# An attention and feed-forward kernel on one core: raw keys and queries loaded once, a third place for the maxima's operands, casts a head sooner

## The reference

```
scores = q @ k.T / 8;  cum = cumsum(maximum(s, 0))
scores = where(j > i, -1e9, scores + minimum(cum[j] - cum[i], 0))
attn   = softmax(scores);  x = attn @ v               # heads side by side: 512 wide
h = relu(x @ w_in)                                    # 512 -> 1024
h = h * sigmoid(conv3(h));  x = h @ w_out             # 3 taps along the positions
u = x + (U @ V mixes the positions of x)              # rank 32
out = u + relu(u @ w_ch1) @ w_ch2                     # 512 -> 2048 -> 512
```

## Time and profile before

| what | value |
|---|---|
| median of 3 runs | 897.69 us (897.37 to 901.75) |
| profiled execution, its own time | 895.65 us |
| its span | 893.8 us |
| PE busy | 852.6 us (95%) |
| DVE busy | 465.5 us (52%) |
| ACT busy | 377.6 us (42%) |
| DMA | 150.36 MB, mean 168 GB/s |
| body 0, attention alone | to about 79 us |
| PE from 820 to 840 us, dense products alone | 153 in 20.00 us, 0.131 each |

### The profile page before, as it was taken

How to read it: one execution, slowest core, us unless ns; L and a number is a source line. 1 busy time by engine, 2 the same in 40 slices (tenths; PEclk the granted TensorE clock), 3 DMA queues, 4 the chain that set the end, 5 groups by cost and what they waited for, 6 DMA issues and landing times.

```text
span 893.8 us, 15677 instructions
## 1 busy us (share of the span) xinstructions
PE 852.6 (95%) x6184; PEld 803.2 (90%) x6184; DVE 465.5 (52%) x976; ACT 377.6 (42%) x717; POOL 50.8 (6%) x105
## 2 busy tenths in 40 slices
PE   4888999989999999999999999999999999999998
PEld 3666889879999899999999999999999999999998
DVE  6788686465447925554444951555323732442222
ACT  2777665553426624554233643444222631221110
POOL 3021000000000000000000000000000000000000
PEclk9999999999999999999999999999999999999999
DMA  6686847638563547536535544435435433364441
GB/s 163 168 231 156 289 128 242 219 72 255 199 206 125 175 156 246 176 112 208 168 137 172 175 129 166 135 131 161 149 142 178 166 141 143 142 223 161 168 162 54
DMA packets 64396, 150.36 MB, mean 168 GB/s; under 512 B 30026, under 2 KB 44362, under 8 KB 51780
## 3 DMA queue, kind: packets, MB, share of 16 engines
q1 hardware_dynamic: 61252, 144.50, 49.2%
q0 software_dynamic: 3072, 4.87, 2.0%
HBM read 119.15 MB, written 30.11 MB: 167 GB/s over the span
## 4 chain that ended last, share of the span: by engine, by line
PE 76%; DVE 12%; ACT 6%; issue 4%; DMA 1%; SPq 1%; DVEq 0%; ACTq 0%; POOL 0%
PE psum L1208 21%; PE psum L1210 20%; PE psum L1209 20%; PE psum L1187 6%; DVE psum L916 2%; PE psum L1134 2%; PE psum L1166 2%; PE psum L1164 2%; DVE work L978 2%; DVE work L981 2%; DVE qb L903 1%; ACT work L760 1%; PE psum L1147 1%; PE psum L1274 1%; PE psum L1171 1%
## 5 line engine op out<-in xcount | busy, mean ns | idle before, releaser
L1208 PE MATMUL psum<-uu_hl,ring 128*128 128x288 f32 x512 | 153.0, 299 | 2.4 <-DVE uu_hl L1016 1.5
L1208 PE MATMUL psum<-r_hl,ring 128*128 128x288 f32 x512 | 153.0, 299 | 0.0
L1210 PE MATMUL psum<-r_hl,ring 128*128 128x288 f32 x512 | 151.2, 295 | 0.0
L1209 PE MATMUL psum<-r_hl,ring 128*128 128x288 f32 x512 | 151.1, 295 | 0.0
L1210 PE MATMUL psum<-uu_hl,ring 128*128 128x288 f32 x512 | 150.9, 295 | 0.0
L1209 PE MATMUL psum<-uu_hl,ring 128*128 128x288 f32 x512 | 150.8, 294 | 0.0
L797 ACT ACTIVATE r_hl<-psum 128x288 fp32r<-128x288 f32 x128 | 52.4, 410 | 179.9 <-PE psum L1210 179.8
L1021 DVE SCALAR_TENSOR_TENSOR r_hl<-psum,r_hl 128x288 fp32r<-128x288 f32 x128 | 58.2, 457 | 134.3 <-ACT r_hl L797 134.2
L1187 PE MATMUL psum<-probs,va 128*65 128x320 f32 (+4 forms) x448 | 107.8, 360 | 7.6 <-ACT probs L699 7.6
L916 DVE CUSTOM_DVE_ANT_0 psum<-psum,key_late 128x512 f32<-128x512 f32 (+4 forms) x160 | 84.7, 564 | 46.5 <-PE psum L1134 45.4
L1033 DVE TENSOR_TENSOR u_acc<-psum,u_acc 128x288 f32<-128x288 f32 x96 | 43.8, 457 | 115.5 <-PE psum L1210 115.5
(11 more groups left out here) (102 smaller groups left out, 1616.0 us busy)
## 6 DMA issues: line engine op xcount, KB each, us to landing
...
```

What stands on the lines that cost most here:

```text
L1208: pe.matmul(o, hi, m_hi, start=start, stop=False)
L1209: pe.matmul(o, hi, m_lo, start=False, stop=False)
L1210: return pe.matmul(o, lo, m_hi, start=False, stop=stop)
```

## The change

What it does:

- The raw keys and queries are loaded once, to partitions 0 to 63. Partition 64 of `kq_raw` holds the rows of sums; the tensor `sums` is gone; `s` is read into `work`.
- `qc` has three buffers too. ACT casts straight into `kc` and `qc` (semaphore `cast`), and `max_scores` waits for these. In body 0 and head (1, 0), listed in ALONE, it does so in step 1, else in steps 2 and 3.
- `kb` and `qb` hold the second copy of the high part and the low part, in exchanged halves. For n = 1 to 10 DVE makes the second copy (`key_parts`, `query_parts`); for others ACT, in steps 0 and 1 of the head before (`second_keys`, `second_queries`).
- In body 0 the heads 0, 2, 4, 6 put their values at another place of PSUM (`out_at`), and the eviction of head h comes in step 0 of head h + 1, between its exponentials. `values` waits for the eviction of n - 2.
- The splits of pairs 0 and 1 of batch 0 go from heads 5 and 7 to head (1, 0); pair 2's normalise and split move by a step.
- Weight splits come one product later on ACT and DVE, and their stores too; in body 0 in step 3. The reciprocals of body 0 go to step 4, the raw loads of later bodies to step 2.
- In `END` one pair of products goes between the two halves of the last `gated`, and one less behind the `wo` products.

The diff, cut and moved 8 columns to the left:

```diff
@@ -121,16 +121,17 @@
 CROWS, KROWS = D + 2, 3 * P // 4 + 1
 kq_raw = sb("kq_raw", [P, 2, 2, S], F32)
+sums = kq_raw[D:D + 1, :, :, :]
 kb = [sb(f"kb{i}", [P, S], F32R) for i in range(2)]
...
 kc = [sb(f"kc{i}", [KROWS, S], F32R) for i in range(KCS)]
-qc = [sb(f"qc{i}", [KROWS, S], F32R) for i in range(2)]
+qc = [sb(f"qc{i}", [KROWS, S], F32R) for i in range(KCS)]
 va = [sb(f"va{i}", [P, NT, P], F32) for i in range(2)]
...
 row_max = sb("row_max", [P, 8], F32R)
-sums = sb("sums", [P, 2, S], F32)
@@ -258,7 +266,14 @@
-COPIED = H + 2
+COPIED = range(1, H + 3)
+def second_place(eng, n, part=None):
+    if n in COPIED:
+        copied.wait(eng, n - COPIED[0], part)
+    else:
+        twice.wait(eng, max(n - len(COPIED), 0), part)
 ATT_STEPS = [(h, g) for h in range(H) for g in range(GROUPS)]
@@ -291,10 +306,12 @@
     fill(1)
-    seq.extend(pair("gated", b, FT - 1))
+    seq.append(("gated", b, 0, FT - 1, 0))
+    fill(ahead - 1)
+    seq.append(("gated", b, 0, FT - 1, 1))
     for d in range(KT):
         seq.extend(pair("wo", b, d))
-    fill(2)
+    fill(3 - ahead)
     if late:
@@ -335,7 +352,7 @@
 PLAN = {a: spread(BESIDE[a], len(ATT_STEPS) - 6 * (a == 1), 6 * (a == 1), a == 1) for a in BESIDE}
-END = order(B - 1, second(B - 2, UNITS // 2, UNITS)) + flat(second(B - 1, 0, UNITS))
+END = order(B - 1, second(B - 2, UNITS // 2, UNITS), 2) + flat(second(B - 1, 0, UNITS))
 END_NORMALISE, END_SPLIT = 5, {0: NPAIR - 2, 6: NPAIR - 1}
@@ -389,9 +406,10 @@
         REFILL.setdefault(before, []).append(key)
-REFILL_NEXT = {SEQ[AT[item] + 1]: keys for item, keys in REFILL.items()}
-STORE_AT = {SEQ[AT[before] + 2]: [q] for (b, q), (_, _, before) in BLOCK.items() if b == 0 and before and q not in EARLY}
+REFILL_HIGH, REFILL_LOW = ({SEQ[AT[item] + x]: keys for item, keys in REFILL.items()} for x in (1, 2))
+STORE_AT = {SEQ[AT[before] + 3]: [q] for (b, q), (_, _, before) in BLOCK.items() if b == 0 and before and q not in EARLY}
@@ -436,11 +454,13 @@
+ALONE = [(0, h) for h in range(H)] + [(1, 0)]
 EVICT_LATE = {(a, h) for a in PLAN for h in range(H - 1)
...
-X_SPLIT = [{(5, 0): 0, (7, 0): 1}, {(5, 0): 0, (7, 0): 1}]
-X_SPLIT_LAST = [{}, {(0, 2): (NPAIR - 2,), (1, 0): (NPAIR - 1,)}, {(0, 0): (NPAIR - 2,), (0, 2): (NPAIR - 1,)}]
+X_SPLIT = {(5, 0): 0, (7, 0): 1}
+X_SPLIT_LAST = [{}, {(0, 0): (0, 1), (0, 3): (NPAIR - 2,), (1, 0): (NPAIR - 1,)}, {(0, 0): (NPAIR - 2,), (0, 2): (NPAIR - 1,)}]
@@ -472,8 +492,8 @@
                 kl_done.wait(sp, n - 2)
-            for half in (0, D):
-                sp.dma_start(kq_raw[half:half + D, i, :, :], kq_t[source(a, h)]).then_inc(raw_in[i].sem, 16)
+                second_place(sp, n - 2)
+            sp.dma_start(kq_raw[0:D, i, :, :], kq_t[source(a, h)]).then_inc(raw_in[i].sem, 16)
@@ -505,7 +525,7 @@
         def attention_step(a, h, g):
-            if g == 0:
+            if g == 2 * (a > 0):
                 load(a, h + 3)
@@ -672,25 +694,37 @@
             raw_in[i].wait(act, n // 2)
+            mm_s.wait(act, n - KCS)
+            act.activation(kc[n % KCS][0:D, :], kq_raw[0:D, i, 0, :], ACT.Copy).then_inc(cast.sem, 1)
+        def second_keys(a, h):
+            n, i = a * H + h, h % 2
+            if n >= B * H or n in COPIED:
+                return
             mm_s.wait(act, n - 2)
-            if n >= COPIED:
-                act.activation(kc[n % KCS][0:D, :], kq_raw[0:D, i, 0, :], ACT.Copy).then_inc(twice.sem, 1)
-            act.activation(kb[i][:, :], kq_raw[:, i, 0, :], ACT.Copy).then_inc(prep_hi.sem, 1)
+            act.activation(kb[i][D:2 * D, :], kq_raw[0:D, i, 0, :], ACT.Copy).then_inc(twice.sem, 1)
...
                 return
-            if n >= COPIED:
-                act.activation(qc[i][0:D, :], kq_raw[0:D, i, 1, :], ACT.Copy, scale=SCALE).then_inc(twice.sem, 1)
-            act.activation(qb[i][:, :], kq_raw[:, i, 1, :], ACT.Copy, scale=SCALE).then_inc(prep_hi.sem, 1)
+            raw_in[i].wait(act, n // 2)
+            mm_s.wait(act, n - KCS)
+            act.activation(qc[n % KCS][0:D, :], kq_raw[0:D, i, 1, :], ACT.Copy, scale=SCALE).then_inc(cast.sem, 1)
+        def second_queries(a, h):
+            n, i = a * H + h, h % 2
+            if n >= B * H or n in COPIED:
+                return
+            mm_s.wait(act, n - 2)
+            act.activation(qb[i][0:D, :], kq_raw[0:D, i, 1, :], ACT.Copy, scale=SCALE).then_inc(twice.sem, 1)
...
             mm_mt.wait(act, n)
-            act.activation(qc[h % 2][KROWS - 1:KROWS, :], psf[0:1, MX:MX + S], ACT.Copy, scale=-1.0).then_inc(mrow.sem, 1)
+            act.activation(qc[n % KCS][KROWS - 1:KROWS, :], psf[0:1, MX:MX + S], ACT.Copy, scale=-1.0).then_inc(mrow.sem, 1)
@@ -700,15 +734,16 @@
             n, m = a * H + h, a * NPAIR + h // 2
-            o, sm = D * (h % 2), D * (1 - h % 2)
+            o = D * (h % 2)
+            out = out_at(n)
             mm_pv.wait(act, n)
...
                 few_in.wait(act, m - 2)
-            act.activation(sums[sm:sm + 1, h // 2 % 2, :], psf[D:D + 1, O0:O0 + S], ACT.Identity, bias=EPS)\
+            act.activation(sums[:, h % 2, h // 2 % 2, :], psf[D:D + 1, out:out + S], ACT.Identity, bias=EPS)\
                .then_inc(evict.sem, 1)
             xl_done.wait(act, m - NPAIR)
-            act.activation(x_raw[o:o + D, h // 2, :], psf[0:D, O0:O0 + S], ACT.Copy).then_inc(evict.sem, 1)
+            act.activation(x_raw[o:o + D, h // 2, :], psf[0:D, out:out + S], ACT.Copy).then_inc(evict.sem, 1)
@@ -718,22 +753,28 @@
                 max_to_row(a, h + 1)
-            if g == 3 and not a:
-                prepare_keys(a, h + 2)
-                prepare_queries(a, h + 2)
-            if g == 4 and (a, h) not in EVICT_LATE:
+            if g == 4 and (a or h == H - 1) and (a, h) not in EVICT_LATE:
                 evict_head(a, h)
...
                 exponentials(a, h, c)
-            if (h, g) in X_SPLIT[a > 0]:
-                x_high(a, X_SPLIT[a > 0][h, g])
+            if g == 1 and (a, h) in ALONE:
+                prepare_keys(a, h + 2)
+                prepare_queries(a, h + 2)
+            if g == 0 and h and not a:
+                evict_head(a, h - 1)
+            if a and (h, g) in X_SPLIT:
+                x_high(a, X_SPLIT[h, g])
             for pair in X_SPLIT_LAST[min(a, 2)].get((h, g), ()):
...
         def then(a, h, g):
-            if g == 2:
+            if g == 0:
+                second_keys(a, h + 1)
+            if g == 1:
+                second_queries(a, h + 1)
+            if g == 2 and (a, h) not in ALONE:
                 prepare_keys(a, h + 2)
-            if g == 3:
+            if g == 3 and (a, h) not in ALONE:
                 prepare_queries(a, h + 2)
...
-        def highs(a, h):
-            n, i = a * H + h, h % 2
-            prep_hi.wait(dve, n, 1)
-            dve.tensor_copy(kc[n % KCS][0:D, :], kb[i][0:D, :].bitcast(F32)).then_inc(copied.sem, 1)
-            prep_hi.wait(dve, n)
-            dve.tensor_copy(qc[i][0:D, :], qb[i][0:D, :].bitcast(F32)).then_inc(copied.sem, 1)
-        def key_low(a, h):
+        def key_parts(a, h):
             n, i = a * H + h, h % 2
...
                 return
-            copied.wait(dve, n, 1) if n < COPIED else prep_hi.wait(dve, n, 1)
-            dve.tensor_tensor(kb[i][0:D, :], kq_raw[0:D, i, 0, :], kb[i][0:D, :].bitcast(F32), ALU.subtract)\
+            cast.wait(dve, n, 1)
+            mm_s.wait(dve, n - 2)
+            if n in COPIED:
+                dve.tensor_copy(kb[i][D:2 * D, :], kc[n % KCS][0:D, :].bitcast(F32)).then_inc(copied.sem, 1)
+            dve.tensor_tensor(kb[i][0:D, :], kq_raw[0:D, i, 0, :], kc[n % KCS][0:D, :].bitcast(F32), ALU.subtract)\
                .then_inc(kl_done.sem, 1)
-        def query_low(a, h):
+        def query_parts(a, h):
             n, i = a * H + h, h % 2
...
                 return
-            prep_hi.wait(dve, n)
-            dve.scalar_tensor_tensor(out=qb[i][D:2 * D, :], in0=kq_raw[D:2 * D, i, 1, :], scalar=SCALE,
-                                     in1=qb[i][D:2 * D, :].bitcast(F32), op0=ALU.mult, op1=ALU.subtract)\
+            cast.wait(dve, n)
+            mm_s.wait(dve, n - 2)
+            if n in COPIED:
+                dve.tensor_copy(qb[i][0:D, :], qc[n % KCS][0:D, :].bitcast(F32)).then_inc(copied.sem, 1)
+            dve.scalar_tensor_tensor(out=qb[i][D:2 * D, :], in0=kq_raw[0:D, i, 1, :], scalar=SCALE,
+                                     in1=qc[n % KCS][0:D, :].bitcast(F32), op0=ALU.mult, op1=ALU.subtract)\
                .then_inc(ql_done.sem, 1)
@@ -941,23 +984,20 @@
         def then(a, h, g):
-            if not a and g == 2 and (h, 0) in X_SPLIT[0]:
-                x_low(a, X_SPLIT[0][h, 0])
-            if a and (h, g) in X_SPLIT[1]:
-                x_low(a, X_SPLIT[1][h, g])
+            if a and (h, g) in X_SPLIT:
+                x_low(a, X_SPLIT[h, g])
             if g == 3 and not a:
-                highs(a, h + 2)
-                key_low(a, h + 2)
-                query_low(a, h + 2)
```

(21 more changed lines are left out.)

70 lines of the change are left out of this document (42 added, 28 removed).

## The result

The changed kernel takes **884.16 us** in the median of six runs (883.47 to 886.38), the kernel before 898.83 us (897.37 to 901.75): ratio 0.9848, 95% interval [0.9825, 0.9871]. That is 1.5% faster. The sign was right.

The account below looks back on a forecast made before the run. The prediction took a serial DVE, ACT, DVE chain to bound the alone heads. Gains of 4.7 (alone stage), 0.2 (transition), 1.9 (mixed bodies) and 1.4 (end) sum to 8.2: 897.69 less 8.2 gives 889.5 us, range 884.5 to 894.5.

Parts of the forecast that it names:

- everything goes: Rival: the mixed bodies' four stalls (4.5 us) go, DVE's four parts take 2.08: 885.6, or 884.8 without U/V wait; chance 0.15.
- Overlap of DVE's parts: Alone heads: four parts take 2.30 us; rival without overlap 2.52, giving 890.8 us, chance 0.24.
- Start: nothing: Kernel start: moved key and query parts and casts fall in DVE's wait for PE's first scores, gaining nothing.
- Head 0's 1.38: First alone head, without weight split: DVE's first maximum at 25.5 instead of 26.88, gain 1.38 us.
- Head 3, a loss of 0.4: Alone head where DVE splits U and V: wait for their load grows from 0.44 to 0.85 us, losing 0.4.
- Head 4: Alone head with a normalise in DVE's loop: 7.46 us instead of 7.93, gain 0.47.
- Two output places ... at nothing: Alone stage: ACT's evictions go behind the exponentials, worth nothing while DVE bounds.
- One raw load for two ... at nothing: 32 DMAs of 288 KB fewer, 6% of all bytes, worth nothing except for head 3.
- Transition: From alone stage to mixed bodies, with DVE's 2.42 us spread sums wait: +0.2 us gain, bounds -1 and +1.
- Mixed bodies: Moved second casts and weight casts shrink four PE stalls by 3.8 us together; half taken, 1.9; bounds -0.9 and 3.8.
- "bare" casts: Mixed bodies: 8 of 42 second casts ahead of an exponential lack ACT idle time, costing 4.7 us if PE waited for each.
- The end: A pair of products ahead of PE's 1.39 us stall at 722.79 gives back 1.4 us.

Follow-up runs that it names:

- late_casts: The changed kernel with batch 0's casts of head h+2 back in step 3 and head 8's first step by the later heads' rule: 897.19 us.
- seconds_old: The changed kernel with a head's second casts again beside its first ones, in steps 2 and 3 of the mixed bodies: 890.57 us.
- end_old: The changed kernel with the end's order as before, both halves of the last gate's product ahead of the pair: 885.27 us.
- weights_old2: Traced rerun of the changed kernel with the mixed bodies' weight splits and stores where they were before: 888.76 us traced, median of both labels 888.2.

## Why the prediction was right, and where it was not

The sign and the mechanism of the alone heads were right; the size was not. By the two profiles the forecast looks close (8.2 for 9.3 us), but that is luck: up to head 10 it had 4.9 (4.7 and 0.2) and 2.3 came, behind that 3.3 (1.9 and 1.4) and 6.9 came. By the medians 14.7 us came for 8.2. The time stands next to the rival "everything goes", and that is chance too: its DVE parts at 2.08 us took 2.43, and two of its four stalls stayed.

- **What bounds, and the loop: right.** DVE's wait for ACT's casts was the alone stage's bound. Heads 1, 2 and 5 take 7.11, 7.16 and 7.01 us (forecast 7.0), head 6 7.56 (7.5 and its reciprocal). late_casts shows that the casts' place is the cause. Head 7, which the sum left out, took 7.01 for 7.84: +0.83.
- **Overlap of DVE's parts: between forecast and rival.** Four parts and what follows take 2.43 us (68.88 to 71.31), forecast 2.30, rival 2.52. Only the step from low part of keys to cast of queries overlaps (0.68 apart, 0.75 long); the others start 0.02 to 0.04 after the end. The Trainium skill, VectorE: DVE Perf Modes, section Two Vector instructions with no wait between them, gives the same pattern: those outputs start in another group of 32 partitions than the last, this one does not. By that rule the trace agrees. Read so, the rule spoke for about 2.4 in this order, and not for the 2.52 that I gave it, since one of the four steps stays within a group. The 0.3 us of waiting for the scores occurred in heads 1, 2 and 5 (0.24) and was covered by the normalise in head 6, both as forecast; the weight split took 1.14 and not 1.2.
- **"Start: nothing": wrong, +1.05.** PE's first product starts at 9.18 us, and no longer at 10.24.
- **Head 0's 1.38: not in this profile.** It took 10.02 us, not 8.0: its start was the longest of all (head 2 at 26.35). In eight later traces with the same program up to there head 2 comes at 23.4 to 24.5, and 24.5 is the forecast's 25.5 less the start's 1.05: head 0 then takes 7.1 to 8.1. Before's own start is known from one trace only, so how much of its 9.42 us for head 0 is such a start stays open.
- **"Head 3, a loss of 0.4": near (0.59; the wait 1.01 for 0.85). Head 4: wrong, -0.26 for +0.47.** Missing was the next late transfer: DVE waits for the first pair's spread sums (0.42 us here, 1.02 and 0.96 in seconds_old and end_old, whose head 4 takes 8.79 and 8.72). The PE pause of 2.22 us and the fall of the clock were not foreseen either, but head 4 is as long without the fall.
- **"Two output places ... at nothing": wrong.** They are worth 1.4 (trace) to 2.8 us (medians). The cover I named, DVE's loop, was only 0.3 us longer than PE's, as the prediction itself worked out; evictions ahead of exponentials use that up.
- **"One raw load for two ... at nothing": open**, between 0 and 6.7 us.
- **Transition: -1.26 from head 9 to 10, for +0.2.** The spread sums wait fell from 2.42 to 0.41 us but came at 91.16, not 88.6: the reciprocal ahead of it waits 1.18 us for its gather, which it did not before, and the x splits stand ahead (PE's pauses of 1.14 and 1.22 at 80.08 and 85.72). The 1.0 that I counted here "by its casts" can be head 7's 0.83, which the list of alone heads left out; counted from head 8 on, the transition is -0.43, within the bounds of -1 and +1. No run undid the moved splits.
- **Mixed bodies: 1.9 forecast, 6.3 measured** (2.31 to 8.62), over my upper bound of 3.8. This was the largest error of the sum. Three of the four listed stalls went or shrank, by 0.74, 1.40 and 0.57 us, and weights_old2 and seconds_old bring them back singly. The fourth and its twin gave 0.14 (1.60 to 1.46), not 0.80. PE's waits from 93 to 700 us, small ones too, fell from 11.3 to some 6.5 us: a moved split frees more than the pauses over 0.7 us that I listed. By the two traces the weights' splits are worth 3.2 us and the second casts' place 3.7 without the clock's fall. Halving the sum for "bare" casts was wrong: PE's waits for exponentials in the bodies fell from 2.5 to 1.0 us.
- **The end: 0.35, not 1.4.** I moved a pair ahead of the stall without asking what the pair itself holds up: the next product waits for its sum, 0.99 us.
- **From the profile to the median.** Before's profiled run had a mean granted clock of 1.000. Of 39 other runs of before, five had that and took 895.4 us in the mean; two at 0.998 took 898.4, twelve at 0.996 897.7, eleven at 0.994 899.9, nine at 0.992 900.5. All six of the changed kernel had 0.998. So some 3 us of the 14.7 between the medians go with falls of the clock that before has in most runs and its profile did not have. That is argued from these means; where the falls are is not shown for before, though seconds_old has one behind the stall of 1.58 that before has too. Another 2 are the long start of after's profile. In numbers: 9.3 between the profiles, 3.2 (898.83 less 895.65) and 2.2 (886.38 less 884.16) make the 14.7.

The single parts, undone, cost 13.0, 6.7, 6.4, 4.1, 2.8 and about 0.35 us, 33 in all against 14.7: they are not a sum. That each takes away a cover that the others need fits late_casts, whose heads are longer than before's, but no pair of parts was undone together. The 6.7 is for a load dearer than the one removed.
